# Attention scores with two products in one matmul, spread over more slots, and weight sums on GpSimd

## The reference, cut to what matters

```python
def sm_attn(qq, kk, vv):                       # scale = 1 / sqrt(64)
    s = scale * np.matmul(qq, kk.transpose(0, 1, 3, 2))
    s = s - np.max(s, axis=-1, keepdims=True)
    a = np.exp(s)
    a = a / (np.sum(a, axis=-1, keepdims=True) + 1e-09)
    return np.matmul(a, vv)
p_packed = sm_attn(p, k, v)                    # first scores: 32 packed rows against 576 keys
out = sm_attn(q, p_packed, p_packed)           # second scores: 576 rows against 32
x = out.transpose(0, 2, 1, 3).reshape(4608, 512)
h = x @ w_in                                   # 512 -> 2048
y = (np.maximum(h, 0) + alpha * np.minimum(h, 0)) @ w_out
g = y @ w_gate
result = (g / (1 + np.exp(-g)) * (y @ w_val)) @ w_down
```

## Time and profile before

| | before |
|---|---|
| median of 3 runs | 1558.52 us (1555.52 to 1558.85) |
| the profiled execution | 1558.1 us, span 1556.3 us |
| instructions | 24850, of which 9328 matmuls |
| busy PE / PEld / DVE / ACT / POOL | 1548.7 / 1435.6 / 1110.5 / 708.1 / 176.7 us |
| first stage, 40 to 690 us: busy DVE / ACT / POOL | 505.1 / 401.9 / 134.3 us of 650 |
| DMA | 294.07 MB, 189 GB/s |

### The profile page before, as it was taken

The page is one execution under the profiler, slowest core; times in us unless marked ns, Lnnn a source line. Parts: engine busy times, 40 slices in busy tenths (PEclk is TensorE's granted clock), DMA queues, the critical chain, the costliest instruction groups (busy, mean ns, idle before and its releaser), DMA issues.

```text
span 1556.3 us, 24850 instructions
## 1 busy us (share of the span) xinstructions
PE 1548.7 (100%) x9328; PEld 1435.6 (92%) x9328; DVE 1110.5 (71%) x1956; ACT 708.1 (45%) x1427; POOL 176.7 (11%) x194
## 2 busy tenths in 40 slices
PE   9999999999999999999999999999999999999999
PEld 6999999999999999999988888888888889999999
DVE  5565669877988779888755686557765685677666
ACT  4565567555765567655522252124422251234223
POOL 2654341000000010023200000000000000000000
PEclk9999999999999999999999999999999999999999
DMA  7443323442544345358466666676676668877866
GB/s 269 131 131 120 91 85 113 137 129 87 166 130 136 113 165 169 102 198 296 161 238 226 217 210 194 228 255 204 176 243 224 216 203 261 306 266 247 285 232 195
DMA packets 134503, 294.07 MB, mean 189 GB/s; under 512 B 13472, under 2 KB 44208, under 8 KB 134384
## 3 DMA queue, kind: packets, MB, share of 16 engines
q1 hardware_dynamic: 122400, 249.74, 49.7%
q0 software_dynamic: 11840, 42.48, 7.1%
q10 hardware_dynamic: 144, 0.26, 0.0%
HBM read 240.53 MB, written 51.90 MB: 188 GB/s over the span
## 4 chain that ended last, share of the span: by engine, by line
PE 96%; DVE 3%; DMA 1%; ACT 0%; issue 0%; DVEq 0%; ACTq 0%
PE acc L1070 14%; PE h L846 10%; PE h L848 10%; PE h L847 10%; PE side L846 9%; PE side L847 9%; PE side L848 9%; PE acc L1074 7%; PE acc L846 5%; PE acc L848 5%; PE acc L847 5%; DVE mixed L1536 1%; PE side L1004 1%; DVE piece L1536 1%; PE side L941 0%; DMA wring<-d_scratch 0%
## 5 line engine op out<-in xcount | busy, mean ns | idle before, releaser
L1070 PE MATMUL acc<-g,w 128*128 128x288 f32 x1792 | 272.8, 294 | 0.0
L1070 PEld LDWEIGHTS acc<-g,w 128*128 128x128 f32 x1792 | 248.9, 188 | 0.0
L1419 ACT ACTIVATE rows_b<-side 128x512 f32<-128x512 f32 (+1 forms) x60 | 33.4, 556 | 285.6 <-PE side L848 285.6
L1211 ACT ACTIVATE g<-floats 128x288 fp32r<-128x288 f32 x192 | 85.4, 445 | 165.0 <-DVE floats L1760 118.3
L1074 PE MATMUL acc<-g,w 128*128 128x288 f32 x896 | 156.2, 296 | 0.0
L846 PE MATMUL h<-attn,mixed 128*128 128x288 f32 x512 | 155.4, 303 | 0.5 <-DVE g L1536 0.5
L848 PE MATMUL h<-attn,mixed 128*128 128x288 f32 x512 | 151.1, 295 | 0.0
L847 PE MATMUL h<-attn,mixed 128*128 128x288 f32 x512 | 151.0, 295 | 0.0
L1074 PEld LDWEIGHTS acc<-g,w 128*128 128x128 f32 x896 | 131.2, 188 | 0.0
L1211 ACT ACTIVATE piece<-floats 128x512 fp32r<-128x512 f32 (+2 forms) x217 | 128.5, 616 | 3.2 <-PE side L848 2.9
L1536 DVE TENSOR_TENSOR g<-floats,g 128x288 fp32r<-128x288 f32 x192 | 87.3, 455 | 48.3 <-ACT g L1211 47.0
(11 more groups left out here) (324 smaller groups left out, 3934.8 us busy)
## 6 DMA issues: line engine op xcount, KB each, us to landing
ring<-w_scratch SPq DMA_DIRECT2D x90, 512.0 KB, 4.4
wring<-d_scratch SPq DMA_DIRECT2D x157, 256.0 KB, 2.9
ring_c<-w_scratch SPq DMA_DIRECT2D x60, 512.0 KB, 4.1
w_scratch<-piece POOLq DMA_DIRECT2D x36, 512.0 KB, 3.9
floats<-w_in SPq DMA_DIRECT2D x64, 256.0 KB, 3.1
ring_b<-w_scratch SPq DMA_DIRECT2D x30, 512.0 KB, 4.9
ring<-d_scratch SPq DMA_DIRECT2D x46, 256.0 KB, 2.9
d_scratch<-piece POOLq DMA_DIRECT2D x42, 256.0 KB, 3.5
```

Source lines behind the costliest of these rows:

```text
L1070: pe.matmul(acc[:, m, 0:CH], w2[:, j, x, m * P:(m + 1) * P], g[:, s % 2, 0, :], start=False, stop=False)
L1211: return nc.scalar.activation(dst, src, ACT.Copy, **kw)
```

## The change

Four parts.

1. **Two products in one matmul.** The weight columns that are zero now hold the low part of the pair's own columns: `p_both` and `pack_both` have high parts in the own 64 columns and low parts in the other 64, `p_alone` and `pack_alone` the high parts with zeros. One matmul with `both` and the operand's high part gives high x high in the own 64 rows of the result and low x high in the other 64; one with `alone` and the operand's low part adds high x low. The other 64 rows must then be added to the own ones, so ScalarE copies them out of PSUM to the own rows in SBUF (`low1`, `low2`) and VectorE adds the own rows from PSUM (`join1`, `join2`). Two pieces can no longer add up in one bank, so each score becomes two, one per piece or half, of 4 matmuls, with a join each. Maximum, exponential and transpose read the sum in SBUF. Batch 0 stays as it was.
2. **Order.** Scores and their joins come first in a slot, ahead of `g` of s + 1. Who writes `side` next waits for `joined`.
3. **Tables.** The helpers are replaced by two tables of slots, FIRST and SECOND, MIX_AT and a new KEEP_AT.
4. **Sums.** `sums` moves from VectorE to GpSimd unchanged; a load into the raw slot of a `g` piece also waits for the fourth sum.

```diff
+FIRST = {
+    1: (6, 7, 8, 9, 12),
+    2: (29, 31, 32, 33, 35),
+    3: (42, 43, 45, 46, 49),
+    4: (83, 84, 86, 87, 89),
...
+SECOND = {
...
+    (3, 1): (80, 82, 0, 82, 83, 89, 93, 94),
...
+MIX_AT = {1: 57, 2: 121, 3: 182}
...
-KEEP_AT = [75, 87, 115, 120, 139, 151, 170, 179, 184, 204, 211, 216, 221, 226, 231, 236, 241, 246]
+KEEP_AT = [74, 86, 115, 122, 132, 156, 171, 178, 185, 196, 207, 213, 222, 227, 231, 236, 240, 245]
...
 for _s in range(SLOTS):
+    for _e in FRONT[_s]:
+        if _e[0] in ("scores1", "scores2"):
+            PLAN.append(_e)
+            PLAN += [j for j in JOIN[_s] if j[0][-1] == _e[0][-1] and j[1:] == _e[1:]]
     if _s + 1 < SLOTS:
         PLAN.append(("g", _s + 1))
-    PLAN += FRONT[_s] + MID[_s]
+    PLAN += [e for e in FRONT[_s] if e[0] not in ("scores1", "scores2")] + MID[_s]
...
             def load(p):
                 if RAW_NO[p] >= RING:
-                    once.wait_ge(*low_of(RAWS[RAW_NO[p] - RING]))
+                    last = RAWS[RAW_NO[p] - RING]
+                    once.wait_ge(*low_of(last))
+                    if last[0] == "g":
+                        once.wait_ge(sums_step, 4 * last[1] + 4)
...
-                once.wait_ge(exp1_done, before(e, "scores1"))
-                once.wait_ge(turn2_done, before(e, "scores2"))
+                once.wait_ge(joined, before(e, "join1") + before(e, "join2"))
+                once.wait_ge(turn2_done, min(1, before(e, "scores2")))
...
                 for c in range(2):
-                    for i in range(2):
-                        p = ("k", b, 2 * half + i)
-                        piece_ready(p)
-                        k = piece(p)
-                        mm = product(scores[:, c, :], hl(lambda x: pP[:, x, half, i, :]),
-                                     hl(lambda x: k[:, x, c * CH:(c + 1) * CH]), i == 0, i == 1)
...
+                    at = slice(c * CH, (c + 1) * CH)
+                    pe.matmul(scores[:, c, :], pP[:, 1, half, i, :], k[:, 0, at], start=True, stop=False)
+                    mm = pe.matmul(scores[:, c, :], pP[:, 0, half, i, :], k[:, 1, at], start=False, stop=True)
                 mm.then_inc(scores1_done, 1)
...
+            def low1(e):
...
+                main, low = own(b, i), own(b, 1 - i)
+                copy(s1[main, half, :].rearrange("p (c n) -> p c n", c=2), scores[low, :, :]).then_inc(low_left, 1)
...
+            def low2(e):
...
                 for i in range(2):
+                    copy(attnF[own(b, i), c, half * CH:(half + 1) * CH], scores[own(b, 1 - i), i, :]
+                         ).then_inc(low_left, 1)
...
+            def join1(e):
+                _, b, half, i = e
+                once.wait_ge(scores1_done, scored(b, half, i))
+                main = own(b, i)
+                once.wait_ge(low_left, lows_by(e))
+                into = s1[main, half, :].rearrange("p (c n) -> p c n", c=2)
+                nc.vector.tensor_tensor(into, scores[main, :, :], into, ALU.add).then_inc(joined, 1)
...
+            def join2(e):
+                _, b, c, half = e
+                for i in range(2):
+                    once.wait_ge(low_left, lows_by(e) - 1 + i)
+                    into = attnF[own(b, i), c, half * CH:(half + 1) * CH]
+                    ins = nc.vector.tensor_tensor(into, scores[own(b, i), i, :], into, ALU.add)
+                ins.then_inc(joined, 1)
```

291 lines of the change are left out of this document (154 added, 137 removed), and 14 rows, old and new, of the table SECOND.

## The result

The changed kernel takes **1577.03 us** (median of 4 runs, 1574.87 to 1577.66) where the kernel before takes 1558.45 beside it: ratio 1.0125, 95% interval 1.0112 to 1.0138. It is slower by some 19 us; I had forecast 9 us faster.

The account below looks back on a forecast made before the run. TensorE's stream of matmuls was taken as the bound. -14.8 us for matmuls, +4.5 at scores and +2 at mixes gave -8.3, called -8.6 with small gains: 1558.1 to 1549.5 us, range 1543.5 to 1557.5.

Parts of the forecast that it names:

- 6.5 us of gaps: TensorE's attention stage: gaps opening in the matmul stream, 4.5 us at crowded scores and 2 us at mixes.
- first place: Scores awaiting joins behind late VectorE work, slots 80 to 84, 143 to 149, 162 to 169: 4.5 us back, 0 to 10.
- second place: Mixes at slots 120 to 136 and 181 to 197, two weight groups beside them on VectorE: 2 us back, 0 to 5.
- A stream of matmuls at 0.1325 us: Both scores on TensorE: 112 matmuls of 288 columns leave, each worth 0.1325 us, together 14.8 us off.
- The joins' durations: VectorE additions 0.75 us (64x576) and 0.45 (64x288), 46 us; ScalarE copies 0.68 and 0.41, 42 us.
- ScalarE's copies hide.: Attention stage: ScalarE is busy 402 of 650 us, so 42 us of copies cost no time.
- the crowds: Three groups of slots where scores and joins meet VectorE's norms, transposes and piece lows: 1.5 us each.
- What was put at nothing: Transposes, as the table of gaps lists them: the forecast counted no gap there.
- Sums on GpSimd: Weight sums moved from VectorE: 0.65 to 0.7 us each for 256 columns, 50 us for all 72.
- GpSimd's contention: VectorE operations with two SBUF inputs lengthen beside GpSimd's sums: 15 us back on VectorE, bounds 0 and 38.
- The rival's mechanism, exclusion: GpSimd shuts out VectorE's two-SBUF operations, 38 us on VectorE instead of 15: no change, 1558.5 us; chance 12%.
- The rival of the join chain: At 39 adjacent pairs each score waits 0.6 us for a sum behind late VectorE work: slower, 1566.7 us; chance 9%.

Follow-up runs that it names:

- b_two: Kernel before without the products low x high of both scores, 112 matmuls fewer and nothing added: 1549.91 us, 0.9953.
- g_no_joins: Changed kernel without any ScalarE copy of a low half or VectorE join, so no score waits for a join: 1562.8 us, 1.0032 to the kernel before.
- d_no_copies: Changed kernel without ScalarE's 84 copies of the low rows; a join takes the PSUM rows alone: 1571.85 us, 1.0098 to the kernel before.

## Why the prediction was wrong, point by point

The prediction had 6.5 us of gaps; there are 34. Gaps by what the late matmul belongs to, us (below zero where starts lie a little closer than the usual distance):

| gaps at | before | b_two | g_no_joins | changed | changed less before | forecast |
|---|---|---|---|---|---|---|
| scores | 0.5 | 1.6 | 1.1 | 15.8 | 15.3 | 4.5 (first place) |
| mixes | 2.4 | 2.4 | 7.3 | 7.3 | 4.9 | 2 (second place) |
| transposes | 0.0 | 0.0 | 4.0 | 6.6 | 6.6 | nothing |
| `h` and `y` | -0.7 | 4.8 | 9.0 | 6.7 | 7.4 | nothing |
| elsewhere | 1.3 | 0.2 | 1.3 | 1.3 | 0.0 | nothing |

- **A stream of matmuls at 0.1325 us, 112 fewer, -14.8 us.** Right as a price and in number; starts within a score are 0.13 us apart (0.21 to 0.24 behind a wait). But the -14.8 was booked in full beside gaps counted for other reasons. `b_two` shows that taking the matmuls away opens 5.7 us of gaps by itself: in slots in which VectorE needs as long as TensorE, a shorter slot gains nothing. I read VectorE's average (505 of 650 us) where its slot by slot sum was needed. This step failed, by some 6 us, and with it the silent assumption that `h` and `y` open no gap.
- **The joins' durations.** Right: 0.743 us for 64x576 and 0.452 for two-input 64x288, estimated 0.75 and 0.45; ScalarE's copies 0.647 and 0.406, estimated 0.68 and 0.41:

```profile
L1748 DVE TENSOR_TENSOR floats<-side,floats 64x288 f32<-64x288 f32 x32 | 14.5, 452 | 3.3 <-ACT floats L1269 2.8
...
L1632 DVE TENSOR_TENSOR floats<-side,floats 64x576 f32<-64x576 f32 x16 | 11.9, 743 | 0.9 <-ACT floats L1269 0.7
```

- **"ScalarE's copies hide."** Wrong: 5 us (`d_no_copies`). The cover in percent was there, the cover in order was not: the copy waits for a score at the head of the slot, what stands behind it waits too, and transposes, scores, `h` and `y` each lose 1 to 2 us.
- **First place, 4.5 us back (0 to 10).** This step failed by the most. The mechanism and the crowds were right: the waits listed on joins at the scores are 9.4 us on L1632, within my 3 to 10. The size was off: 15.8 us of gaps at scores, 15.3 more than before, of which `g_no_joins` takes 14.7 away. Three crowds at 1.5 us each stood in my sum; slots 82 to 84 alone have 2.5 us, from 480 to 560 us there are 5.0 us at five scores, and gaps lie outside the crowds too (1.84 us before the score at 353.71, 1.18 before 363.93). The claim that the table had moved the maxima out of the way was read off the slots' numbers; the rows above show maximum and subtraction standing between two joins, as the order listing ahead of the prediction did.
- **Second place, 2 us back (0 to 5).** Too small: 4.9 us more at mixes, at the upper end of the range. I looked at VectorE's work in two stretches of mixes and costed only what was added in microseconds, not what comes ahead of what. The longest gap of the changed kernel is there, 2.95 us before the mix at 609.46. In VectorE's queue a norm and its transpose, the low part of `g`, three low parts of pieces and a combining stand ahead of the two low parts of the mix:

```profile
602.44 0.76 DVE L1784 TENSOR_TENSOR floats<-floats 128x576 f32<-128x576 f32 x1
603.23 0.78 DVE L1788 STREAM_TRANSPOSE floats<-floats 128x576 f32<-128x576 f32 x1
603.93 0.88 DVE L1610 TENSOR_TENSOR g<-floats,g 128x288 fp32r<-128x288 f32 x1
604.73 2.70 DVE L1610 TENSOR_TENSOR piece<-floats,piece 128x512 fp32r<-128x512 f32 x3
607.47 0.51 DVE L1825 SCALAR_TENSOR_TENSOR floats<-floats,h 128x288 f32<-128x288 f32 x1
608.01 1.39 DVE L1610 TENSOR_TENSOR mixed<-side,mixed 64x512 fp32r<-64x512 f32 x2
```

  GpSimd's four sums run from 602.84 to 606.55; beside them `g` takes 0.88 and the three pieces 2.70 us, where the means of those that meet none are 0.45 and 3 x 0.69. So contention lengthens this very chain by about 1 us, though the move of the sums helps in all.
- **What was put at nothing: transposes, 6.6 us.** The exponential stands between the last join and the transposes. With each half's score in two slots it comes later, and for batches 2 and 4 the new table has it one slot ahead of the transposes (slots 34 and 35, 88 and 89), where the old helpers had it two ahead (33 and 35, 87 and 89). Just there transposes wait for it, 1.3 and 1.7 us; a third long wait, 1.6 us at 188.3, is for a join of the second attention. I read this off table and trace and did not move a slot to test it; without joins 4.0 of the 6.6 us remain. The chain of batch 4, each step late by what stands before it (VectorE, ScalarE, TensorE):

```profile
310.20 0.75 DVE L1637 TENSOR_REDUCE floats<-floats 128x1 f32<-128x576 f32 x1
```

```profile
310.98 0.77 ACT L1375 ACTIVATE floats<-floats 128x576 f32<-128x576 f32 x1 [0.89 <-DVE floats L1637]
```

```profile
311.90 0.44 PE L1002 MATMUL side<-floats 128*128 128x128 f32 x2 [1.69 <-ACT floats L1375]
```

- **Sums on GpSimd, 0.65 to 0.7 us each.** Too low in all: means of 0.84 to 1.08 by place and operand, 67 us and not 50. The size by itself was nearly right: the ten sums that meet no VectorE operation with two SBUF inputs took 0.73 to 0.74 us. The rest, some 14 us, is what the meetings cost GpSimd, which I had not counted.

```profile
L861 POOL TENSOR_TENSOR floats<-floats 128x256 f32<-128x256 f32 x12 | 10.1, 838 | 85.8 <-DMA floats<-w_val 83.2 <-PE side L1002 2.5
...
L861 POOL TENSOR_TENSOR late_sums<-floats 128x256 f32<-128x256 f32 x6 | 6.5, 1084 | 1.1 <-DVE piece L1610 1.1
```

- **GpSimd's contention, 15 us on VectorE.** It exists and is larger. Summing what VectorE operations that overlap a GpSimd one take above their mean alone gives 28 to 30 us from 45 to 810 us, where the kernel before has 4; half of it (some 14 us in 25 operations) is on `g`; the `g` row of the same stretch as the earlier trace rows went from 449 to 474 ns:

```profile
L1610 DVE TENSOR_TENSOR g<-floats,g 128x288 fp32r<-128x288 f32 x133 | 63.1, 474 | 20.3 <-ACT g L1269 19.1
```

  Operations with an input in PSUM show no excess. The rival's mechanism, exclusion, is what the rows show (last section); the price is below its 38 us because not every sum meets such an operation and because GpSimd is the one that waits where VectorE begins first. In sum the move still helped the changed kernel (5.5 us), so that rival (1558.5) does not explain the loss; what contention by itself costs there stays open.
- **The rival of the join chain (1566.7, 9%).** It had the right sign and the right place. It asked for 39 waits of 0.6 us; there are 17 of 0.9 on average, 15.8 us in all, just over the 15 from which I had said it would hold (9.4 by the list of waits). Put into my sum in place of the 4.5, the measured 15.8 gives 1560.8, still 16 us short: no rival had the gaps at transposes, `h` and `y`. That was the real gap in the list of cases: each took one mechanism and held all else at its estimate.
- **What stays open.** 14 us belong to joins and copies, shown. The other 20 of the 34 us of gaps are shown to be there without joins, and by place of wait (mixes 5, transposes 4, `h` and `y` 10). 5.7 us of gaps come from the missing matmuls alone in the old slots (`b_two`), and 5.3 from the move of the sums in the old slots, but that move has the other sign in the new ones. Among the tables it does not split: kept pieces cost the kernel before 13.6 us by themselves, and undone together with the mixes give the changed one 0.9, within what the runs tell apart. No slots were found here in which the new form pays.

## What to carry to other kernels

When an in-order engine is late now and then, price a change of its list by walking the list slot by slot with running lateness, not by busy time over a stretch: in this stage engines busy for 82% and 67% (531 and 436 of 650 us) made TensorE wait 34 us. A wait placed at the head of a slot (a copy for a score, a sum for a load) delays everything that the engine's order puts behind it. And removing work from the bounding engine returned its full price here only where the next engine had room in those very slots; a kernel that only leaves the work out (`b_two`) gives that bound in one run, and here it was half the gain on paper.
